# One table-driven instruction for the two shares of a lone query, and one guard instruction for two tiles

## The reference

```python
q_bits = (np.einsum('bhsd,dk->bhsk', q, proj) > 0).astype(np.int64)
k_bits = (np.einsum('bhsd,dk->bhsk', k, proj) > 0).astype(np.int64)
...
mask = q_bucket[:, :, :, None] == k_bucket[:, :, None, :]
scores = scale * np.matmul(q, k.transpose(0, 1, 3, 2))
scores = np.where(mask, scores, -1000000000.0)
scores = scores - np.max(scores, axis=-1, keepdims=True)
attn = np.exp(scores)
attn = attn / (np.sum(attn, axis=-1, keepdims=True) + 1e-09)
return np.matmul(attn, v).astype(np.float32)
```

## Time and profile before

| | us |
|---|---|
| median of 3 runs | 672.41 |
| lowest and highest | 672.07, 672.5 |
| the profiled execution, its span | 670.8 |
| what lies around the span (672.4 less 670.8) | 1.6 |
| TensorE busy | 663.7 |
| VectorE busy | 495.9 |
| ScalarE busy | 346.6 |
| GpSimd busy | 474.2 |

### The profile page before, as it was taken

The page is one execution under the profiler, slowest core; times in us unless marked ns, Lnnn a source line. Parts: engine busy times, 40 slices in busy tenths (PEclk is TensorE's granted clock), DMA queues, the critical chain, the costliest instruction groups (busy, mean ns, idle before and its releaser), DMA issues.

```text
span 670.8 us, 11966 instructions
## 1 busy us (share of the span) xinstructions
PE 663.7 (99%) x3892; PEld 576.8 (86%) x3892; DVE 495.9 (74%) x976; ACT 346.6 (52%) x761; POOL 474.2 (71%) x538
## 2 busy tenths in 40 slices
PE   8999999999999999999999999999999999999998
PEld 6776777777777699999999999988898988989896
DVE  6878878788788799869778963678877666555554
ACT  6887777877777630011103453555545554454433
POOL 6774756788876899968870528799987776777710
PEclk9999999999999999999999999999999999999999
DMA  6673836638352111111110201212232124212102
GB/s 159 152 161 102 192 88 155 151 88 187 91 132 75 34 32 32 32 32 33 32 40 25 95 1 33 79 48 80 79 93 64 64 78 143 64 64 65 45 18 94
DMA packets 58492, 54.17 MB, mean 81 GB/s; under 512 B 28640, under 2 KB 47488, under 8 KB 58432
## 3 DMA queue, kind: packets, MB, share of 16 engines
q1 hardware_dynamic: 56784, 53.02, 29.2%
q10 hardware_dynamic: 1648, 0.39, 0.3%
HBM read 32.51 MB, written 3.15 MB: 53 GB/s over the span
## 4 chain that ended last, share of the span: by engine, by line
PE 88%; POOL 6%; issue 2%; ACT 1%; DVE 1%; DMA 1%; DVEq 0%; ACTq 0%; POOLq 0%
PE psO L1544 10%; PE psS L1522 10%; PE psR L1530 9%; PE psR L1628 7%; PE psR L1627 7%; PE psR L1629 7%; PE psS L1627 6%; PE psS L1628 6%; PE psS L1629 6%; PE psS L1730 4%; PE psS L1729 4%; PE psS L1728 4%; POOL w_lo L736 3%; PE psR L1470 1%; POOL w_raw L727 1%
## 5 line engine op out<-in xcount | busy, mean ns | idle before, releaser
L577 POOL TENSOR_SCALAR probs<-probs,lone,inv 128x768 f32<-128x768 f32 x96 | 93.9, 985 | 58.6 <-DVE inv L1145 58.5
L736 POOL TENSOR_TENSOR w_lo<-w_raw,w_hi 128x256 fp32r<-128x256 f32 x96 | 79.2, 838 | 44.6 <-ACT w_hi L982 43.9
L1128 DVE TENSOR_REDUCE neg_max<-psS 128x1 f32<-128x768 f32 x96 | 91.2, 950 | 12.9 <-PE psS L1522 8.7
L803 ACT ACTIVATE probs<-psS,neg_max 128x768 f32<-128x768 f32 x96 | 86.5, 901 | 15.7 <-DVE neg_max L1128 15.6
L560 POOL TENSOR_SCALAR w_hi<-w_raw 128x256 fp32r<-128x256 f32 (+1 forms) x79 | 49.0, 624 | 50.2 <-PE psS L1629 28.9
L812 ACT ACTIVATE probs_t<-psR 128x384 f32<-128x384 f32 x131 | 60.7, 491 | 31.2 <-PE psR L1530 30.7
L1530 PE MATMUL psR<-ident,probs 128*128 128x128 f32 x576 | 74.6, 273 | 0.4 <-POOL probs L577 0.2
L1530 PEld LDWEIGHTS psR<-ident,probs 128*128 128x128 f32 x576 | 66.5, 140 | 5.5 <-POOL probs L577 2.1
L1544 PE MATMUL psO<-probs_t,v_raw 128*64 128x384 f32 x384 | 68.8, 494 | 0.0
L1379 DVE TENSOR_TENSOR v_raw<-psR,early 128x384 f32<-128x384 f32 x64 | 35.3, 552 | 32.4 <-PE psR L1629 32.2
L1384 DVE TENSOR_TENSOR v_raw<-v_raw,bits 128x384 f32<-128x384 f32 x64 | 53.7, 841 | 6.7 <-ACT bits L1005 4.3
(11 more groups left out here) (275 smaller groups left out, 1881.5 us busy)
## 6 DMA issues: line engine op xcount, KB each, us to landing
w_raw<-in_moe_w_in SPq DMA_DIRECT2D x16, 512.0 KB, 3.4
w_raw<-in_moe_w_out SPq DMA_DIRECT2D x32, 256.0 KB, 2.7
w_raw<-in_moe_w SPq DMA_DIRECT2D x9, 512.0 KB, 3.8
h_lo<-w_hi SPq DMA_DIRECT2D x22, 192.0 KB, 3.3
h_hi<-w_hi SPq DMA_DIRECT2D x18, 192.0 KB, 3.4
w_raw<-in_q SPq DMA_DIRECT2D x16, 192.0 KB, 3.6
v_raw<-in_v SPq DMA_DIRECT2D x16, 192.0 KB, 2.5
stacks<-w_hi SPq DMA_DIRECT2D x16, 192.0 KB, 3.3
```

The source lines that it names most:

```text
L577: pool.tensor_scalar(probs[i % PROBS][:, :], probs[i % PROBS][:, :], lone[:, i % 6:i % 6 + 1], inv[:, i % 6:i % 6 + 1], ALU.add, ALU.mult) ...
L736: pool.tensor_tensor(in2_slot(w_lo, n, which), in2_raw(n, PARTS2[which]), f32(in2_slot(w_hi, n, which)), ALU.subtract).then_inc(in2_split, 1)
L803: act.activation(probs[i % PROBS][:, :].rearrange("p (a b) -> p a b", a=2), psS[i % 2][:, :, 0:HALF], ACT.Exp, bias=neg_max[:, i % 6:i % 6 ...
L1128: dve.tensor_reduce(neg_max[:, i % 6:i % 6 + 1], psS[i % 2][:, :, 0:HALF], AX.XY, ALU.min).then_inc(max_ready, 1)
```

## The change

`lone` and `lone_sums` become the two halves of one tile `shares`. A table `lone_share` with 2^60 in its first two columns and 768 * 2^60 in the other two is set once, by two memsets. Both halves then come from one instruction, which compares the negated maximum (read twice, through a broadcast) and multiplies by the table. The guard of two tiles is one instruction instead of two, with the shares as its second tensor instead of as a scalar for each partition. The semaphore counts follow. `shares` takes the place of both old tiles, and `lone_share` is new, so each tile allocated behind them lies 32 bytes further on in every partition.

```diff
-        lone = sb("lone", [P, 6], F32)
-        lone_sums = sb("lone_sums", [P, 6], F32)
+        shares = sb("shares", [P, 2, 6], F32)
+        lone_share = sb("lone_share", [P, 2, 2], F32)
...
-                pool.tensor_scalar(probs[i % PROBS][:, :], probs[i % PROBS][:, :], lone[:, i % 6:i % 6 + 1],
+                pool.tensor_scalar(probs[i % PROBS][:, :], probs[i % PROBS][:, :], shares[:, 0, i % 6:i % 6 + 1],
                                    inv[:, i % 6:i % 6 + 1], ALU.add, ALU.mult).then_inc(probs_normed, 1)
...
-                dve.tensor_scalar(lone[:, cols], neg_max[:, cols], MASKED / 2, LONE, ALU.is_ge, ALU.mult).then_inc(lone_found, 1)
-                dve.tensor_scalar(lone_sums[:, cols], neg_max[:, cols], MASKED / 2, S * LONE, ALU.is_ge,
-                                  ALU.mult).then_inc(lone_found, 1)
+                if i == 0:
+                    dve.wait_ge(share_set, 2)
+                dve.scalar_tensor_tensor(shares[:, :, cols], neg_max[:, cols].unsqueeze(1).broadcast_to([P, 2, count]), MASKED / 2,
+                                         lone_share[:, :, 0:count], ALU.is_ge, ALU.mult).then_inc(lone_found, 1)
                 dve.wait_ge(probs_ready, i + count)
-                dve.wait_ge(lone_found, 2 * inverted(i))
-                for c in range(i % 6, i % 6 + count):
-                    dve.tensor_scalar(guarded[:, c:c + 1], sums[:, c:c + 1], 1e-9, lone_sums[:, c:c + 1], ALU.add,
-                                      ALU.add).then_inc(sums_guarded, 1)
-                dve.wait_ge(sums_guarded, i + count)
+                dve.wait_ge(lone_found, inverted(i))
+                dve.scalar_tensor_tensor(guarded[:, cols], sums[:, cols], 1e-9, shares[:, 1, cols], ALU.add,
+                                         ALU.add).then_inc(sums_guarded, 1)
+                dve.wait_ge(sums_guarded, inverted(i))
                 dve.reciprocal(inv[:, cols], guarded[:, cols]).then_inc(inv_ready, 1)
...
+            dve.memset(lone_share[:, 0, :], LONE).then_inc(share_set, 1)
+            dve.memset(lone_share[:, 1, :], S * LONE).then_inc(share_set, 1)
```

More of the change, by code:

```diff
@@ L269, in lsh_attention_ffn @@
         probs_ready = sem("probs_ready")
+        share_set = sem("share_set")
         lone_found = sem("lone_found")
```

## The result

| | before | after |
|---|---|---|
| median, us | 672.24 (672.04 to 672.5, 4 runs) | 680.26 (679.82 to 680.51, 4 runs) |
| the profiled execution: span | 670.8 | 677.9 |
| what lies around the span, run by run | 1.76 to 1.86 (58 runs of before in the comparisons below) | 2.10 to 2.13 (4 runs) |
| VectorE instructions | 976 | 882 |

The ratio is 1.0119, with a 95% interval from 1.0104 to 1.0133. The kernel got 8.0 us slower with 94 VectorE instructions fewer; the prediction said 680.8. (One profiled execution further down, of the version with the new instructions in the pair chains, ran at a granted clock of 0.56 from end to end and took 1100 us; nothing is read from it.)

What follows compares the result with a forecast made beforehand. TensorE was taken to bound the kernel, so only waits or the stage's start and end could matter. 4.4 + 1.9 + 1.3 + 1.1 - 0.3 = 8.4 us gave 680.8 us; range 674.5 to 687 (0.80).

Steps and rivals of the forecast that it cites:

- filling: Attention stage up to 30 us: TensorE already waits for exponentials, so lateness passes through; 1.1 us, bounds 0 and 2.9.
- projection groups: Second turn group of pairs 1 to 6: late row maximum stalls TensorE 0.73 us, six times, 4.4 us.
- groups with sums: Groups with three GpSimd sums of x: shares and guard wait, late normalisations stall TensorE 0.64 us, three times, 1.9 us.
- carried on: Groups 20 to 22 and from 24: remaining sums cover shares and guard, lateness enlarges the next stall by 0.65, twice, 1.3 us.
- end of the stage: Normalisations of tiles 93 and 94: GpSimd covers little, so the shorter chains gain the whole 0.29; -0.3 us.
- The premise: VectorE instructions reading two SBUF tensors, as the new ones do, can't start until GpSimd's current instruction ends.
- The walk through the turn groups: Groups 17 and 18: shares wait for GpSimd's subtraction L573, so the row maximum starts 0.48, then 1.08 us late.
- What the pair chain gives back: Chain for two tiles: one guard instead of two shortens it from 0.34 to 0.16 us, returning 0.18 us.
- A: Rival: the new instructions don't wait for GpSimd, only the end of the stage gains; 672.1 us, chance 0.12.
- B: Rival: they wait, but TensorE has more slack; six stalls of 0.4 to 0.73, little else; 674.5 to 677.5 us, chance 0.13.
- C: Rival: VectorE is passed over at seams of GpSimd's work, 1.0 us per miss, five to ten; 685 to 691 us, chance 0.10.
- D: Rival: faster, since fill and end together hold 1 to 3 us of waits; chance 0.02.

Runs made afterwards that it cites:

- The last run: The changed kernel with old forms back in the pair chains (two tiles), new instructions only in the single chains (one tile): 684.77 us, ratio 1.0184 to before.
- the bare forms: A kernel of its own, computing nothing of the reference: nine small VectorE instructions, each started beside long and short GpSimd instructions; no whole-kernel time given.

## Why the prediction was right, term by term

| term of the sum | predicted | measured |
|---|---|---|
| filling | 1.1 | 0.80 (group 3; 0.77 and 0.78 in the two executions of the same code) |
| projection groups, six | 6 x 0.73 = 4.4 | 6 x 0.52 = 3.1 |
| groups with sums, three | 3 x 0.64 = 1.9 | 0.69 + 0.70 + 0.67 = 2.1 |
| carried on, twice | 2 x 0.65 = 1.3 | 0.70 + 0.69 = 1.4 |
| memsets and 32 bytes | 0 | 0.4 drift |
| end of the stage | -0.3 | -0.29 |
| sum at the end of the stage | 8.4 | 7.5 |

The measured steps are differences of neighbouring groups in the lateness. The projection steps of pairs 1 to 4 are 0.53, 0.51, 0.52 and 0.52; those of pairs 5 and 6 are 0.73 and 0.76, of which I book 0.52 as projection and the rest (0.21, 0.24) as carried on, with the steps in groups 20 and 21 (0.27 + 0.22) and in 24 and 25 (0.27 + 0.18).

*The premise* was right in the kernel and by itself. *The price alone* was right: 0.16 for the guard (138.32), and the fastest `shares` 0.152.

*The walk through the turn groups* was right almost to the hundredth on the way in. In group 17 the row maximum should be 0.48 late; TensorE was 2.64 late there, so 128.80 - 125.72 - 2.64 = 0.44. In group 18 it should be 1.08; 136.32 - 132.67 - 2.66 (the mean of 2.64 and 2.68) = 0.99.

*What the pair chain gives back* is the term that was mis-sized. I took 0.18, the difference of the guards (0.34 against 0.16). From the start of the guards to the marks it was 135.27 - 134.67 = 0.60 us before and 138.63 - 138.32 = 0.31 after: 0.29 given back. That takes 0.11 off each stall, and the 0.09 less at the row maximum comes on top: 0.73 - 0.11 - 0.09 = 0.53, and 0.52 was measured. Six times 0.21 is the 1.3 us by which the projection term was too high. The last run shows that the same term acts in the first turn group too.

*The sums groups* went as written: the third L626 covered the guard, and TensorE waited for the normalisations; 0.69 for 0.64. *Carried on* was an estimate of 1.3 and measured 1.4. I had left open that the new instructions might slip into the seams. They did so with the guard alone, but not here, since the new `shares` moved the guard onto the third sum.

*The fill* was 0.80 for 1.1, within its bounds. It needs both halves of the change: the shares alone cost 0.28 there, the guard alone nothing, the pair chains nothing. The share that its two kinds of waits have in it (for exponentials 2.9 to 3.8, for normalisations 0.9 to 1.3 us) was not separated.

*The end* gave 0.29, as said.

*Around it:* 7.5 us at the end of the stage became 7.1 in the span. This is not the change: nearly all the other kernels' profiled executions also gain 0.3 to 0.5 us on that of before behind the stage (the one with the 32 bytes is 0.42 late at group 32, and its span is 0.04 shorter), so before's own profiled execution was that much long there. Its span is 670.8, and the median of 58 spans of before is 670.4. The 1.6 us around the span that the prediction took over were a median (672.4) less the span of that one execution. Run by run, 1.76 to 1.86 us lie around it before, and 2.08 to 2.18 in all 22 runs of the kernel after and of the three versions that keep the whole change. So 0.3 us of the loss lie outside the span, and the prediction had no term for them. All 49 runs of the kernels before with an edit, and of those with a part of the change, have 1.76 to 1.86; what makes the difference is open. Median spans 7.7 apart (678.1 against 670.4) and 0.3 around them are the 8.0. That the forecast of 680.8 came within 0.6 was thus partly luck: a stage sum 0.9 too high met 0.3 around the span, 0.2 within it and a before that was 0.2 faster than in the prediction (672.24 against 672.4). Inside the stage sum, too, 0.4 of drift that it had at nothing stood against 1.3 too much for the projection groups.

*The rivals.* A: gone by the bare forms. B: the stalls in the projection groups are 0.52, inside its 0.4 to 0.73, but "little else" was wrong. C: no `shares` or `guarded` instruction took over 1.65 us, and the longest, at 31.58, ends at 33.23, where the L574 that it started beside ends at 33.21; each of the long ones ends within 0.03 of the end of the GpSimd instruction that it met, so none was passed over at a seam. In the chances, the range to 687 holds a third of C's 685 to 691 and not almost half, 0.03 instead of 0.04. D: the end gave 0.3, nothing else did. Of the signs that I named, one was weak: TensorE's busy share hardly fell, as the waits stood inside modelled matmuls. The staircase of starts showed what the busy share hid.

## What to carry to other kernels

On VectorE, the form of a small instruction counts for more than how many there are: two inputs in SBUF, or two columns with immediates, make it wait for whatever long instruction GpSimd has begun, and a one-column form with a scalar for each partition passes. Before fusing small steps, look at what GpSimd runs beside them and at what stands behind them in VectorE's queue. Where a chain must use such a form, put it behind the row maximum that TensorE waits for, if its own consumer has lead; that recovered 6.0 of 8.0 us here, and cost 1.0 where there was no lead (3.0 over before against 2.0). And compare starts of the same work in both traces, group by group: busy shares don't show where time went. Take in one start that stands ahead of the change, since it differed by up to 0.4 us between executions of the same code.

## What the runs showed of the hardware beyond that

Sixteen bytes per partition of unused tile, which move every later tile by 32 bytes, made the same program drift: against before, the starts of TensorE's products moved from -0.09 (group 3, all of it there at the first row maximum) to +0.43 (group 31). Every version with the 32 bytes shows that drift (0.02 to 0.04 per group where nothing else happens), and the two versions without them (guard only, and before with the moved chain) do not. The groups by line from 60 to 220 us have it in the score matmuls, first before, then with the 32 bytes:

```profile
L1522 PE MATMUL psS<-h_lo 128*128 128x384 f32 (+1 forms) x72 | 17.0, 358 | 0.0
```

```profile
L1523 PE MATMUL psS<-h_lo 128*128 128x384 f32 (+1 forms) x72 | 17.2, 360 | 0.0
```

That is 0.1 to 0.2 us in each of the four groups of score matmuls. What in the addresses does it is open, and in the whole time it is too small to be told from no change.

On GpSimd's side the wait needs no second input: a scaling of 0.83 us held VectorE's two-input form as the subtraction did. And a reciprocal over two columns passes (0.15 us) where a multiplication by an immediate over two columns waits (1.47).

Not tried in the kernel: the passing form with its first input in PSUM. It would need the table or the sums in PSUM. The four score banks, the three of the ring and the one of the products each use 384 of 512 columns in this stage; whether the rest would do is open.
